# Both MLPs' first layers by seven products of halves: fused attention and two MLPs on one core

## What is computed

```python
def _attn_ref(q, k, v):                       # (4, 8, 576, 64)
    # means of 4 neighbours, full softmax attention over 144 of them, repeated 4 times
    out_d = sm_attn(q_d, k_d, v_d); out_up = np.repeat(out_d, 4, axis=2)
    # plus attention under the mask |i - j| < 4
    out_local = np.matmul(softmax(where(mask, scale * q @ k.T, -1e9)), v)
    return out_up + out_local

def _moe_ref(x, w_gate, w_val, w_out):        # (2304, 512), (512, 1536) twice, (1536, 512)
    gate = 1.0 / (1.0 + np.exp(-(x @ w_gate)))
    return gate * (x @ w_val) @ w_out

def _moe2_ref(x, w_in, w_out):                # (2304, 512), (512, 2048), (2048, 512)
    h = x @ w_in
    return (h * (1.0 / (1.0 + np.exp(-1.702 * h)))) @ w_out
```

## Time and profile before

| | us |
|---|---|
| median of 3 runs | 965.17 (964.18 to 965.36) |
| the profiled execution, its own time | 965.12 |
| its span, first to last instruction | 963.3 |
| PE busy | 949.9 (99%) |
| DVE, ACT, POOL busy | 471.9, 250.8, 211.8 |

### The profile page before, as it was taken

The page is one execution under the profiler, slowest core; times in us unless marked ns, Lnnn a source line. Parts: engine busy times, 40 slices in busy tenths (PEclk is TensorE's granted clock), DMA queues, the critical chain, the costliest instruction groups (busy, mean ns, idle before and its releaser), DMA issues.

```text
span 963.3 us, 16170 instructions
## 1 busy us (share of the span) xinstructions
PE 949.9 (99%) x6926; PEld 893.9 (93%) x6926; DVE 471.9 (49%) x787; ACT 250.8 (26%) x598; POOL 211.8 (22%) x135
## 2 busy tenths in 40 slices
PE   8999999999999999999999999999999999999998
PEld 6777899999999999999999999999999999999997
DVE  5777435343343353343333365655555554646544
ACT  5777531111111111111111122222222222222221
POOL 5667235030030030030024460202020201101000
PEclk9999999999999999999999999999999999999999
DMA  9865201010010010010010001100001010100013
GB/s 312 254 192 146 83 1 66 1 66 1 1 66 1 1 66 1 1 36 9 1 44 1 1 1 45 42 3 12 33 1 44 1 44 1 45 1 1 1 69 129
DMA packets 14120, 43.86 MB, mean 46 GB/s; under 512 B 1760, under 2 KB 1760, under 8 KB 12384
## 3 DMA queue, kind: packets, MB, share of 16 engines
q1 hardware_dynamic: 14048, 42.82, 13.3%
HBM read 38.10 MB, written 4.72 MB: 44 GB/s over the span
## 4 chain that ended last, share of the span: by engine, by line
PE 97%; DVE 1%; issue 1%; ACT 0%
PE s_ps L346 26%; PE d_ps L346 26%; PE t_ps L346 22%; PE o_ps L346 15%; PE o_ps L319 1%; PE d_ps L271 1%; PE t_ps L331 1%; PE d_ps L279 1%; PE t_ps L304 1%; PE o_ps L339 1%; DVE o_tok L603 1%; PE s_ps L258 1%; PE t_ps L292 1%; PE s_ps L247 0%; PE t_ps L397 0%
## 5 line engine op out<-in xcount | busy, mean ns | idle before, releaser
L660 DVE TENSOR_TENSOR g_lo<-g_raw,g_hi 128x384 fp32r<-128x384 f32 x168 | 138.7, 825 | 97.4 <-ACT g_hi L523 97.4
L346 PE MATMUL s_ps<-x_hi,w_hi 128*128 128x384 f32 x480 | 161.1, 336 | 0.1
L346 PE MATMUL s_ps<-x_hi,w_lo 128*128 128x384 f32 x480 | 161.0, 335 | 0.0
L346 PE MATMUL s_ps<-x_lo,w_hi 128*128 128x384 f32 x480 | 160.7, 335 | 0.0
L346 PE MATMUL d_ps<-x_hi,w_hi 128*128 128x384 f32 x480 | 160.5, 334 | 0.0
L346 PE MATMUL d_ps<-x_hi,w_lo 128*128 128x384 f32 x480 | 160.3, 334 | 0.0
L346 PE MATMUL d_ps<-x_lo,w_hi 128*128 128x384 f32 x480 | 160.3, 334 | 0.0
L658 DVE TENSOR_TENSOR g_raw<-sig,s_ps 128x384 f32<-128x384 f32 x84 | 46.6, 554 | 219.7 <-ACT sig L521 219.6
L521 ACT ACTIVATE sig<-s_ps 128x384 f32<-128x384 f32 x84 | 41.3, 492 | 420.1 <-PE s_ps L346 420.1
L734 POOL CAST w_hi<-w_raw 128x2048 fp32r<-128x2048 f32 (+1 forms) x13 | 29.3, 2252 | 552.0 <-PE o_ps L346 551.9
L523 ACT CAST g_hi<-g_raw 128x384 fp32r<-128x384 f32 x168 | 86.2, 513 | 130.8 <-DVE g_raw L658 130.8
(11 more groups left out here) (101 smaller groups left out, 1428.5 us busy)
## 6 DMA issues: line engine op xcount, KB each, us to landing
w_raw<-in_w_two_dram SPq DMA_DIRECT2D x8, 1024.0 KB, 4.7
w_raw<-in_w_one_dram SPq DMA_DIRECT2D x5, 1536.0 KB, 6.7
vw<-in_v_win_dram SPq DMA_DIRECT2D x32, 170.6 KB
vt<-in_v_tok_dram SPq DMA_DIRECT2D x16, 320.0 KB, 4.3
qk<-in_q_t_dram SPq DMA_DIRECT2D x16, 288.0 KB, 4.2
qk<-in_k_t_dram SPq DMA_DIRECT2D x16, 288.0 KB, 5.0
out_dram<-y SPq DMA_DIRECT2D x18, 256.0 KB, 2.1
w_raw<-in_w_one_dram SPq DMA_DIRECT2D x3, 512.0 KB, 6.1
```

The source lines that it names most:

```text
L346: mm = pe.matmul(bank, a, b, start=(i == 0), stop=(i == len(steps) - 1))
L660: vec.tensor_tensor(g_lo[:, n % 2, f, :], g_raw[:, f, :], g_hi[:, n % 2, f, :], ALU.subtract).then_inc(g_ready, 1)
```

## The change

Let a product of two 2-by-2 block matrices be computed with seven block products instead of eight (the form with four sums of the left and four of the right operand, `S1` to `S4` and `T1` to `T4`). The halves are those of the 512 inputs, of a group's 256 features, and of 768 tokens. The tokens go through in three thirds (`PASS` = 768), each with all groups of a layer: six phases, (layer 1, third 0), (1, 1), (2, 0), (1, 2), (2, 1), (2, 2). There are 42 groups now, 18 in layer 1 and 24 in layer 2, and a weight block `b` for each 256-by-512 matrix of a group: two in layer 1 (gate, value), one in layer 2, 60 in all. Weights are loaded and split anew in each phase.

- PE: a `product` is six matmuls of 384 columns; `p1` to `p7` accumulate into three banks of a block's set. Between them ACT copies a bank's state to SBUF (`snap_p1`, `snap_u2`, `snap_u3`) and DVE adds it to another bank (`c11`, `c22`, `c12`). Second products (`second`) have two banks in `o_ps` for all their blocks. The order is written out for each kind of neighbouring groups.
- The gated values stay in PSUM: DVE's product writes into the bank of the value, and `g_hi`, `g_lo` are made from there.
- POOL computes the four sums of a weight block (256 elements a partition each, `sums_in_begin`, `sums_in_end`) and of a third's tokens (768 each, `sum_t1` to `sum_t4`), and all subtractions for the `_lo` parts. ACT rounds: `round_in`, `round_in_sums`, `round_out`, `round_x`. What the next phase needs of `x` is spread over the groups of this one (`x_step`, `round_x_step`).
- SP loads a block with 512 KB into the one `w_raw` when the block before has been split (`wa_ready`), and a group's second-layer weights, 512 KB, into one of two `v_raw`, whose earlier contents must have been used (`y_ready`). `att` takes the place of `y`, and is stored by thirds.
- In the attention `add_levels` cuts a unit at 768 tokens, so that eight units have three pieces instead of two.

The diff, cut to its core:

```diff
+PASS = 2 * NT
+NPASS = TOK // PASS
 FG = 2
-G1, G2 = FF1 // (FG * P), FF2 // (FG * P)
-N1, N2 = G1 * TILES, G2 * TILES
-NN = N1 + N2
-OB1 = DM // P
-OB2 = NT // P
-W1 = 3 * FG * DM
-W2 = 2 * FG * DM
-YT = KC * NT
-WP = 512
-SPLITS = W1 // WP
-WL = FG * DM
+WG = FG * P
+NP = 7
...
+        x_bank = [s_ps[:, 0, 0:NT], d_ps[:, 1, 0:NT]]
+        y_bank = [s_ps[:, 1, 0:NT], t_ps[:, 0, 0:NT]]
+        z_bank = [d_ps[:, 0, 0:NT], t_ps[:, 1, 0:NT]]
...
+            def load_in(b):
+
+                if b >= 1:
+                    sp.wait_ge(wa_ready, b)
+                k, m = BLOCKS[b]
+                q, lay, p, g = GROUPS[k]
+                sp.dma_start(w_raw[:, :, :].rearrange("p a n -> p (a n)"), w_gate_val[g, m] if lay == 1 else w_in2[g]
+                             ).then_inc(w_loaded, 16)
+
+            def load_out(k):
+                q, lay, p, g = GROUPS[k]
+                if k >= 2:
+                    sp.wait_ge(y_ready, y_count(k - 1))
+                sp.dma_start(v_raw[k % 2][:, :, :].rearrange("p a n -> p (a n)"), w_out1[g] if lay == 1 else w_out2[g]
+                             ).then_inc(v_loaded[k % 2], 16)
+
...
+            load_out(1)
+            load_in(2)
+            load_in(3)
+            for k in range(NG):
+                if k >= 1 and k + 1 < NG:
+                    load_out(k + 1)
+                if k + 2 < NG:
+                    load_in(FIRST[k + 2])
+                    if layer(k + 2) == 1:
+                        load_in(LAST[k + 2])
+                for q in (2, 4):
+                    if k == START[q + 1] + 1:
+                        store(q)
+            store(5)
...
+            def product(b, bank, w, x, start):
+
+                wh, wl = w_hi[b % 2], w_lo[b % 2]
+                q = GROUPS[BLOCKS[b][0]][0]
+                xh, xl = xs_hi[q % 2], xs_lo[q % 2]
+                for c in range(2):
+                    cols = slice(c * P, (c + 1) * P)
+                    pe.matmul(bank, wh[:, w, cols], xh[:, x, c, :], start=(start and c == 0), stop=False,
+                              skip_group_check=True)
+                    pe.matmul(bank, wh[:, w, cols], xl[:, x, c, :], start=False, stop=False, skip_group_check=True)
+                    mm = pe.matmul(bank, wl[:, w, cols], xh[:, x, c, :], start=False, stop=(c == 1), skip_group_check=True)
+                mm.then_inc(in_done[b % 2], 1)
...
+            def p7(b):
+                wait_x(b, 5)
+                pe.wait_ge(u2_ready, b + 1)
+                product(b, x_bank[b % 2], S3, T3, False)
...
+            def from_one_to_one(k):
+
+                v, n, w = LAST[k], FIRST[k + 1], LAST[k + 1]
+                p1(n)
+                p4(v)
+                p2(n)
+                p3(v)
+                p6(n)
+                p5(n)
+                second(k, 0)
+                p7(n)
+                second(k, 1)
+                second(k, 2)
+                p4(n)
+                second(k, 3)
+                p3(n)
+                second(k, 4)
+                p1(w)
+                second(k, 5)
+                p2(w)
+                p6(w)
+                second(k, 6)
+                p5(w)
+                p7(w)
+                second(k, 7)
...
+            def from_two_to_two(k):
+                n = FIRST[k + 1]
+                p1(n)
+                second(k, 0)
+                p2(n)
+                p6(n)
+                second(k, 1)
+                p5(n)
+                p7(n)
+                second(k, 2)
+                p4(n)
+                second(k, 3)
+                p3(n)
+                second(k, 4)
+                second(k, 5)
...
+            def round_in(b):
+
+                act.wait_ge(w_loaded, 16 * b + 16)
+                if b >= 2:
+                    act.wait_ge(in_done[b % 2], NP * (b // 2))
+                nc.scalar.copy(w_hi[b % 2][:, A11:A22 + 1, :], w_raw[:, R11:R22 + 1, :]).then_inc(wahi_ready, 1)
+
+            def round_in_sums(b):
+                act.wait_ge(wsum_ready, b + 1)
+                nc.scalar.copy(w_hi[b % 2][:, S1:S4 + 1, :], w_sum[b % 2][:, S1:S4 + 1, :]).then_inc(wshi_ready, 1)
...
+            def snap_u2(b):
+                act.wait_ge(in_done[b % 2], NP * (b // 2) + 3)
+                if b >= 1:
+                    act.wait_ge(c12_ready, b)
+                nc.scalar.copy(u2_sb[:, :], x_bank[b % 2]).then_inc(u2_ready, 1)
...
+            def next_first(k):
+
+                if k + 2 < NG:
+                    round_in(FIRST[k + 2])
+                    round_in_sums(FIRST[k + 2])
...
+            def from_one_to_one(k):
+                n, w = FIRST[k + 1], LAST[k + 1]
+                snap_p1(n)
+                hi22(k)
+                hi21(k)
+                sig11(k + 1)
+                snap_u2(n)
+                hi12(k)
+                round_in(w)
+                round_in_sums(w)
+                snap_u3(n)
+                sig22(k + 1)
+                sig21(k + 1)
+                round_out(k + 1)
+                round_x_step(k)
+                sig12(k + 1)
+                snap_p1(w)
+                next_first(k)
+                snap_u2(w)
+                hi11(k + 1)
+                snap_u3(w)
...
+            def from_two_to_two(k):
+                n = FIRST[k + 1]
+                snap_p1(n)
+                next_first(k)
+                sig11(k + 1)
+                snap_u2(n)
+                hi11(k + 1)
+                round_out(k + 1)
+                round_x_step(k)
+                snap_u3(n)
+                sig22(k + 1)
+                hi22(k + 1)
+                sig21(k + 1)
+                hi21(k + 1)
+                sig12(k + 1)
+                hi12(k + 1)
...
+            def c11(b):
+                dve.wait_ge(in_done[b % 2], NP * (b // 2) + 2)
+                dve.wait_ge(p1_ready, b + 1)
+                vec.tensor_tensor(y_bank[b % 2], p1_sb[:, :], y_bank[b % 2], ALU.add).then_inc(c11_ready, 1)
...
+            def gate(k, n, f, t, bank):
+                dve.wait_ge(sig_ready[n], k + 1)
+                values = bank[LAST[k] % 2]
+                vec.tensor_tensor(values, sig[:, t, f, :], values, ALU.mult).then_inc(gated[n], 1)
+
+            def low(k, n, f, t, bank):
+                dve.wait_ge(ghi_ready[n], k + 1)
+                vec.tensor_tensor(g_lo[k % 2][:, t, f, :], bank[LAST[k] % 2], g_hi[k % 2][:, t, f, :], ALU.subtract
+                                  ).then_inc(g_ready[n], 1)
...
+            def from_two_to_two(k):
+                n = FIRST[k + 1]
+                add_up(k, 0)
+                c11(n)
+                gate11(k + 1)
+                add_up(k, 1)
+                low11(k + 1)
+                c22(n)
+                add_up(k, 2)
+                gate22(k + 1)
+                add_up(k, 3)
+                gate21(k + 1)
+                low22(k + 1)
+                c12(n)
+                low21(k + 1)
+                add_up(k, 4)
+                gate12(k + 1)
+                add_up(k, 5)
+                low12(k + 1)
...
+            def sums_in_begin(b):
+                raw, into = w_raw, w_sum[b % 2]
+                pool.wait_ge(w_loaded, 16 * b + 16)
+                if b >= 2:
+                    pool.wait_ge(in_done[b % 2], NP * (b // 2))
+                sum_in(b, S1, raw[:, R21, :], raw[:, R22, :], ALU.add).then_inc(wsum_step, 1)
+                pool.wait_ge(wsum_step, 2 * b + 1)
+                sum_in(b, S2, into[:, S1, :], raw[:, R11, :], ALU.subtract).then_inc(wsum_step, 1)
+
+            def sums_in_end(b):
+                raw, into = w_raw, w_sum[b % 2]
+                sum_in(b, S3, raw[:, R11, :], raw[:, R21, :], ALU.subtract)
+                pool.wait_ge(wsum_step, 2 * b + 2)
+                sum_in(b, S4, raw[:, R12, :], into[:, S2, :], ALU.subtract).then_inc(wsum_ready, 1)
+
+            def low_in(b):
+                pool.wait_ge(wahi_ready, b + 1)
+                gp.tensor_tensor(w_lo[b % 2][:, A11:A22 + 1, :], w_raw[:, R11:R22 + 1, :], w_hi[b % 2][:, A11:A22 + 1, :],
+                                 ALU.subtract).then_inc(wa_ready, 1)
+
+            def low_in_sums(b):
+                pool.wait_ge(wshi_ready, b + 1)
+                gp.tensor_tensor(w_lo[b % 2][:, S1:S4 + 1, :], w_sum[b % 2][:, S1:S4 + 1, :], w_hi[b % 2][:, S1:S4 + 1, :],
+                                 ALU.subtract).then_inc(ws_ready, 1)
+
+            def split_in(b):
+                sums_in_begin(b)
+                sums_in_end(b)
+                low_in(b)
+                low_in_sums(b)
+
+            def low_out(k):
+                pool.wait_ge(vhi_ready, k + 1)
+                gp.tensor_tensor(v_lo[k % 2][:, :, :], v_raw[k % 2][:, :, :], v_hi[k % 2][:, :, :], ALU.subtract
+                                 ).then_inc(v_ready, 1)
...
+            def x_step(k):
+
+                q = GROUPS[k][0] + 1
+                step = k - START[q - 1]
+                if q == len(PHASES):
+                    return
+                quarter = parts(PHASES[q][1])
```

(89 more changed lines are left out.)

717 lines of the change are left out of this document (550 added, 167 removed).

## The result

The changed kernel takes **1010.0 us** (median of 4 runs, 1007.7 to 1011.1) against 965.3 us: ratio 1.0464, 95% interval 1.0437 to 1.0491. (One of the four executions of the kernel before took 3325.6 us; the other three have a median of 965.2.) I had forecast 970 with a range of 945 to 992. The direction was right, the time lies 40 us off and outside the range. The profiled execution took 1009.07 us with a span of 1007.0.

What follows compares the result with a forecast made beforehand. PE was taken to bound the kernel, busy 99% of the span. Span 963.3 - 62.4 + 56.7 + 8.0 + 0.5 + 2.5 = 968.6, plus 1.8 above span, so 970 us; range 945 to 992.

Steps and rivals of the forecast that it cites:

- What goes, 62.4 us: PE, both layers: seven products instead of eight remove 360 matmuls of 0.1733 us each, saving 62.4 us.
- Layer 1 hides everything: Layer 1's 18 groups: other engines' work costs nothing above PE's slots, 22.9 us a group, margins 1.2 us or more.
- the rival that the lock holds every DVE operation: Layer 1, DVE beside POOL: `low21` would wait up to 2.4 us against 1.8 of slack; no chance given.
- The wait in layer 2, 56.7 us: Layer-2 groups, PE ahead of p7: 2.7 us wait for block landing, sums and ACT's queue, 21 times, adding 56.7 us.
- the subtraction's slope: POOL's sums of 256 elements: this pricing gave 0.74 us each; the forecast took 0.63, near the additions.
- x casts ahead of p4, 8.0 us: Four steps of two layer-2 phases: `round_x_step` before `snap_u3` delays PE, 1.2 us (three steps) or 0.4 (one), 8.0 us.
- Attention and start, 3.0 us: Attention's extra `add_levels` pieces cost 0.5 us; at layer 1's start PE waits 2.5 us before `p1(2)`.
- The clock, taken as unchanged: PE, whole kernel: clock expected to stay 1.00, since attention's short idle pieces keep it there.
- my rival: Clock falls after each layer-2 stand, three products at half speed: 21 x 3.5 = 73 us, time 1043; chance 0.03.
- a wait above 2.45 us: Layer-2 groups, ahead of p7: break-even wait, 2.45 us in each of 21; the sign hangs on it.

Runs made afterwards that it cites:

- the last version: Changed kernel with both casts of the next block behind `snap_u3` and ACT's and POOL's order at layer 1's start altered: 907.2 us, ratio 0.9399.
- the run that held the clock: Changed kernel with 26 needless PE matmuls of 128 columns ahead of p7 in each of 21 layer-2 groups: 986.3 us, ratio 1.0218.
- 1.4 us of filling: Changed kernel with 14 needless PE matmuls of 128 columns ahead of p7 in each of 21 layer-2 groups: 998.2 us, ratio 1.0329.
- 1.5 to 1.9 of standing alone: Changed kernel with the block's load before the second-layer weights' load, both still waiting for the previous group's second products: 960.5 us, ratio 0.9940.

## Why the prediction was wrong, step by step

- **What goes, 62.4 us.** Right: 360 matmuls less, and cadences of 0.173 and 0.231 us in the changed kernel too. The span of the last version is 905.3, or 963.3 - 58.0; most of the missing 4.4 us is the attention's 0.8, the stand of 0.57 and the 2 us of small excesses that the kernel before doesn't have.
- **Layer 1 hides everything.** Right: no gap from 130 us to the end of that phase, PE busy 239.97 of 240 us, with POOL at 87%. DVE's products and subtractions with one input in PSUM took 0.55 to 0.56 us each beside it, so the rival that the lock holds every DVE operation is out. One reading was loose: the subtraction in the earlier trace rows ended 0.4 us behind the POOL instruction, not with it.
- **The wait in layer 2, 56.7 us.** The mechanism, place and count were right (21 times, ACT's `snap_u2` behind the block's landing); the term measured 64.2. Landing came 0.1 later than forecast, in two groups 1.5 (once SP took 1.44 us to issue the load instead of 0.43, once six stores were on their way beside it), and POOL's sums took 0.74 each, not 0.63. That error was a choice: I placed them near the attention's additions and not by the subtraction's slope, which had given 0.74.

```profile
L1304 POOL TENSOR_TENSOR w_sum<-w_raw 128x256 f32<-128x256 f32 x120 | 88.6, 738 | 224.5 <-DMA w_raw<-in_w_in_dram 184.7
```

The Trainium skill ("GPSIMD Engine Reference", reconciling with measured numbers) gave an estimated 0.7 by its slope, and the measurement agrees with it better than with my number.
- **x casts ahead of p4, 8.0 us.** Right in size where the clock was held: six pairs of 1.05 us (I had 1.2), and 0.3 to 0.4 for the single cast (0.4), which my limit of 0.5 us had put among the slow matmuls. In the changed kernel two pairs show, 2.1 us, and one single cast (731.34 us); the rest was hidden by the slow clock.
- **Attention and start, 3.0 us.** 0.8 (the attention's last copy `p_t` comes at 108.50 us instead of 107.72) and 3.6. The place was wrong: PE stood at p7 of block 1, not at p1 of block 2, since ACT's `snap_u2(1)` is queued behind `round_in_sums(2)`. It is the same pattern as in layer 2, and I had overlooked it there.
- **The clock, taken as unchanged.** This is the step that failed. "No row shows a gap of 2.7", so I gave the clock 3 in 100 and priced it at 73 us. It cost 34.9 us as I added it up, some 30 of them at half clock: 16 of the 21 stands brought a slow stretch, and 14 of those cost 1.5 to 2.0 us, where my rival had 3.5 for each. With 963.3 - 62.4 + 64.2 + 2.1 + 34.9 + 3.6 + 0.8 = 1006.5 the span of 1007.0 is accounted for. Without the clock's 30 us and with the 5 us of x casts that it hid the same sum gives an estimated 982 and a time of 984, inside the range, and the run that held the clock measured 986.3. The direction came out right for the stated reason, a wait above 2.45 us (3.06 measured), with no help from the clock. The rows of the attention speak of short pauses only, and couldn't bear a chance that low for 21 stands of 2.7 us, which my own sum contained. The Trainium skill ("TensorE: Matmul & The Clock Gate", HAM oscillation) describes a loop in which a wait for transfers in each round sends the array back to 1.2 GHz; the trace agrees in kind (0.50 of full clock behind the stands). A mechanism that multiplies a wait belonged in the forecast with more than a token chance.

What stays open is which stands the clock answers. In the changed kernel stands of 2.8 to 3.5 us were followed by half clock 14 times and five times (2.8 to 3.0 us) not at all. With 1.4 us of filling and mostly 1.3 to 1.7 of standing it was 13 of 21. With 1.5 to 1.9 of standing alone it was none of 20, and with 26 filling matmuls and little standing none of 21. So neither the length of the stand nor the time since the last matmul of the program itself sorts the cases; no run here shows what does.

## What to carry to other kernels

A wait that one's own sum puts into PE's queue many times over has to be priced at both levels of the clock: here 64 us of standing brought some 28 us of matmul time at half clock with it, and taking 1.3 us off a landing gave back 49 us. In a design that hands PE's partial results through another engine in order (the snapshots here), nothing that waits for a transfer may stand ahead of them in that engine's queue; moving two casts by six places turned +4.6% into -5.5%, and with the start mended -6.0%. Walk every in-order queue for its last arrival before counting on what an algorithm with fewer matmuls saves.

## What the runs showed that I had not expected

- POOL's fp32 addition of contiguous operands costs 0.738 us for 256 elements and 1.84 for 768, 2.15 ns an element, as its subtraction with a rounded result does; the attention's additions run at 1.66 ns an element. Why is open.
- A slow stretch costs much the same each time, 1.5 to 2.0 us, whether 1.4 or 3.1 us of standing stood before it, and 2.6 to 2.8 behind the two of 4.3 us.
- Needless matmuls can pay: 26 in each of 21 groups made the kernel 23.7 us faster, though removing the waits they filled gained 97.
